# A token list built in bf16, a rotated loop body on VectorE, and moved weight splits in a two-layer expert kernel on one core

## The reference

```
x = soft_moe(x)                      # x = c @ slot_out: each token is a mix of 32 slots
logits = x @ w_gate;  noise_scale = log1p(exp(x @ w_noise))
noisy = logits + noise_scale * noise
top2 = two largest of noisy;  top2_w = softmax over the two
for e in range(E):
    for k in range(2):
        mask = top2[:, k] == e
        h = maximum(x[mask] @ w1[e], 0)
        out[mask] += top2_w[mask, k] * (h @ w2[e])
```

## Time and profile before

| | us |
|---|---|
| median of 3 runs | 1197.89 (1194.05 to 1198.15) |
| the profiled execution | 1196.62 |
| its span, first to last instruction | 1194.8 |
| mean granted PE clock | 0.843 of full speed |

### The profile page before, as it was taken

How to read it: one execution, slowest core, us unless ns; L and a number is a source line. 1 busy time by engine, 2 the same in 40 slices (tenths; PEclk the granted TensorE clock), 3 DMA queues, 4 the chain that set the end, 5 groups by cost and what they waited for, 6 DMA issues and landing times.

```text
span 1194.8 us, 18812 instructions
## 1 busy us (share of the span) xinstructions
PE 958.0 (80%) x5371; PEld 741.2 (62%) x5371; DVE 885.5 (74%) x1882; ACT 414.0 (35%) x758; POOL 666.7 (56%) x817
## 2 busy tenths in 40 slices
PE   4778887888877878787877787857669999999896
PEld 3666665666666666666666675215357877777785
DVE  7999999999999999999999983025444434443432
ACT  3444444444444444444444431110322212221220
POOL 2777777777777777777777751004024444443433
PEclk7888788777788788888788878966779999998998
DMA  9811011011011011011011006999305434423333
GB/s 353 335 41 42 1 42 41 0 41 41 0 41 41 0 41 41 0 41 41 0 41 41 0 1 228 380 421 425 145 10 109 89 55 108 108 29 37 37 38 37
DMA packets 21583, 105.15 MB, mean 88 GB/s; under 512 B 2944, under 2 KB 4016, under 8 KB 12464
## 3 DMA queue, kind: packets, MB, share of 16 engines
q1 hardware_dynamic: 13696, 84.55, 18.1%
q0 software_dynamic: 7136, 11.22, 7.6%
q10 hardware_dynamic: 720, 9.00, 2.0%
HBM read 88.40 MB, written 16.09 MB: 87 GB/s over the span
## 4 chain that ended last, share of the span: by engine, by line
issue 39%; PE 27%; DVE 26%; DMA 4%; DVEq 2%; ACT 1%; POOL 0%; POOLq 0%; SPq 0%; PEldq 0%
PE psum L738 11%; DVE arena L904 9%; DVE arena L900 8%; PE psum L743 5%; DVE arena L893 5%; DMA arena<-w_soft 2%; DMA arena<-xs_rows,arena 2%; PE psum L727 2%; PE psum L698 1%; PE psum L641 1%; PE psum L712 1%; PE psum L534 1%; PE psum L688 1%; DVE h_lo L1139 1%; DVE arena L919 1%
## 5 line engine op out<-in xcount | busy, mean ns | idle before, releaser
L900 DVE MATCH_REPLACE8 arena<-arena 128x576 f32<-128x576 f32 x432 | 316.6, 739 | 0.0
L904 DVE MAX8 arena<-arena 128x8 f32<-128x576 f32 x432 | 303.8, 743 | 0.0
L501 PE MATMUL psum<-arena 128*128 128x128 f32 x576 | 130.2, 367 | 150.3 <-POOL arena L1190 150.2
L1184 POOL TENSOR_SCALAR arena<-arena 128x576 bf16<-128x576 f32 x142 | 244.5, 1731 | 6.6
L486 PE MATMUL psum<-arena 128*128 128x288 f32 x576 | 222.5, 550 | 4.6 <-DMA arena<-qkv 4.6
L514 PEld LDWEIGHTS psum<-arena 128*128 128x128 f32 (+3 forms) x1600 | 193.4, 182 | 30.1 <-issue 3.5
L514 PE MATMUL psum<-arena 128*128 128x65 f32 (+3 forms) x1600 | 207.5, 271 | 0.9 <-ACT arena L782 0.9
L501 PEld LDWEIGHTS psum<-arena 128*128 128x128 f32 x576 | 82.5, 180 | 183.0 <-POOL arena L1190 155.8
L486 PEld LDWEIGHTS psum<-arena 128*128 128x128 f32 x576 | 153.2, 280 | 53.6 <-DMA arena<-qkv 4.6
L1190 POOL TENSOR_TENSOR arena<-arena 128x576 f32<-128x576 f32 x142 | 178.5, 1278 | 0.0
L781 ACT COPY arena<-psum 128x512 f32<-128x512 f32 x144 | 84.2, 585 | 231.3 <-PE psum L502 231.3
(11 more groups left out here) (173 smaller groups left out, 971.4 us busy)
## 6 DMA issues: line engine op xcount, KB each, us to landing
weights<-w_soft SPq DMA_DIRECT2D x21, 1024.0 KB, 16.9
arena<-qkv SPq DMA_DIRECT2D x15, 1189.0 KB, 5.3
weights<-w_top SPq DMA_DIRECT2D x12, 1024.0 KB, 27.4
arena<-w_soft SPq DMA_DIRECT2D x11, 1024.0 KB, 11.6
weights<-w_top SPq DMA_DIRECT2D x3, 2048.0 KB, 21.8
weights<-w_top ACTq DMA_DIRECT2D x3, 2048.0 KB, 8.0
out<-arena SPq DMA_DIRECT2D x1, 4864.0 KB, 18.9
arena<-w_top SPq DMA_DIRECT2D x4, 1024.0 KB, 27.8
```

Of the source, the lines that this page charges most:

```text
L501: nc.tensor.transpose(bank(4 + t % 2, P, c * P), src[:, c * P:(c + 1) * P], ident)
L900: nc.vector.match_replace(work[t % 2], m8[t % S_SLOTS][:, 8 * r - 8:8 * r], src, NEG) \
L904: nc.vector.max(m8[t % S_SLOTS][:, 8 * r:8 * r + 8], work[t % 2]) \
L1184: nc.gpsimd.tensor_scalar(keep[t % 2], s_sb[t % S_SLOTS], m8[t % S_SLOTS][:, TOPK - 1:TOPK], None, ALU.is_ge) \
```

## The change

What it does:
- **The list** is built from bf16 one-hot matrices, exact for the small whole numbers in it, by 36 single-pass matmuls with 94 columns: 47 that add up which of the 36 blocks a row is in, and 47 that add up (partition - 128), made by ACT. POOL makes the first 47, DVE the compare (`col_hot`) and all of `onehot` in three parts. A few DVE operations turn the two sums into a row index and an output row for each place; `list_i` holds both.
- **Tokens from the list**: the 33rd word of a row is gone. An output row is numbered by partition and block rather than by token, and the host puts the rows in the order of tokens at the end. The scatter takes its rows from the list's second word; the copies L1128 and L1147 and the counters `x_free` and `tok_set` go. `fetch` copies both words ahead of the scatter.
- **The gate weights** are worked out earlier on DVE, and POOL instead of DVE multiplies the rows by them.
- **Loop body on DVE rotated**: y of tile i - 1 is taken out at the start of tile i's body. `w2_low(e + 2)` thereby stands between c_low of an expert's last tile and y of that tile.
- **Weight splits** are made in halves; ACT's `w2_high` runs one expert further ahead; `w2_low(1)` stands behind `c_low(1)`, ahead of the first y.
- **G stacks**: eight stacks use six pairs of banks; experts 6 and 7 are taken out only after expert 0's tiles; PE's first f_trans waits for the first six.
- **Bounds**: each engine loads all nine at once ahead of the loop.

The diff, cut to its core (constants, semaphores and layout are left out):

```diff
-        G_BANKS = [(3, 4), (0, 5)]
+        G_BANKS = [(3, 4), (0, 5), (3, 4), (0, 5), (1, 2), (6, 7), (3, 4), (0, 5)]
...
+        def tile_bounds(eng):
+            return [eng.value_load(tab[0:1, e:e + 1], min_val=min(e, 1), max_val=TILES) for e in range(E + 1)]
...
             def g_stack(e):
                 pe.wait_ge(g_lo, 2 * (e // 4) + 2)
-                if e >= 2:
-                    pe.wait_ge(g_ev[0], e - 1)
-                    pe.wait_ge(g_ev[1], e - 1)
+                if e in (2, 3, 6, 7):
+                    last_user = max(n for n in range(e) if G_BANKS[n] == G_BANKS[e])
+                    pe.wait_ge(g_ev[0], last_user + 1)
+                    pe.wait_ge(g_ev[1], last_user + 1)
                 for x in range(2):
                     for n, part_ in enumerate((gq_hi, gq_lo)):
                         first = (1 - n) * SL
-                        last = nc.tensor.matmul(bank(G_BANKS[e % 2][x]), pick[:, e % 4, first:first + P],
+                        last = nc.tensor.matmul(bank(G_BANKS[e][x]), pick[:, e % 4, first:first + P],
                                                 part_[:, x * BANK:(x + 1) * BANK], start=(n == 0), stop=(n == 1))
                     last.then_inc(g_rep, 1)
 
             g_group(0)
 
-            pe.wait_ge(hot_hi, 1)
+            pe.wait_ge(hot_act, 1)
+            pe.wait_ge(hot_pool, 1)
             for a in range(PICKS):
-                if a % 14 == 0:
-                    pe.wait_ge(*((hot_dve, a // 14 + 1) if a < 28 else (hot_pool, 1)))
-                last = nc.tensor.matmul(bank(B_X, COLS), onehot[:, a, :], hi_hot[:, a, :],
+                if a % 12 == 0:
+                    pe.wait_ge(hot_dve, a // 12 + 1)
+                last = nc.tensor.matmul(bank(B_X, 2 * COLS), onehot[:, a, :],
+                                        hi_hot[:, a, :, :].rearrange("p v q -> p (v q)"),
                                         start=(a == 0), stop=(a == PICKS - 1))
             last.then_inc(list_ps, 1)
             pe.wait_ge(pick_set, 1)
@@ -714,11 +715,14 @@
                 last.then_inc(f_t, 1)
 
             pe.wait_ge(rt_ready, 1)
-            pe.wait_ge(idx_ready, 1)
+            bounds = tile_bounds(pe)
+            pe.sem_inc(f_y, 1)
+            pe.wait_ge(g_ev[0], 6)
+            pe.wait_ge(g_ev[1], 6)
             f_trans(16)
             for e in range(E):
-                t0, t1 = first_tile(pe, e), end_tile(pe, e)
-                pe.wait_ge(w_lo, e + 1)
+                t0, t1 = bounds[e], bounds[e + 1]
+                pe.wait_ge(w_lo, 2 * e + 2)
                 pe.wait_ge(g_ev[0], e + 1)
...
-                nc.scalar.copy(w2_hi[e % 4], w2t_of(e % 4)).then_inc(w_hi, 1)
+                for f in (0, FC // 2):
+                    nc.scalar.copy(w2_hi[e % 4][:, f:f + FC // 2, :], w2t_of(e % 4)[:, f:f + FC // 2, :]).then_inc(w_hi, 1)
 
...
             nc.scalar.copy(pick, more[:, M_PICK:MW].rearrange("p (q w) -> p q w", q=4)).then_inc(pick_set, 1)
-            act.wait_ge(rows_set, 2)
-            act.dma_start(xs_dram[0:2 * N, :].rearrange("(p a) r -> p (a r)", a=PICKS), rows_f).then_inc(tabled, 16)
+            act.wait_ge(hot_set, 1)
+            nc.scalar.activation(hi_hot[:, :, 1, :], col_hot, ACT.Copy, scale=cst[:, C_BACK:C_BACK + 1]).then_inc(hot_act, 1)
+            act.wait_ge(rows_set, 1)
+            act.dma_start(xs_dram[0:ROWS, :].rearrange("(p a) r -> p (a r)", a=PICKS),
+                          rows_f).then_inc(tabled, 16)
             g_high(0)
             for e in range(4):
                 g_out(e)
             g_high(1)
             w2_high(0)
-            for e in range(4, E):
+            for e in range(4, 6):
                 g_out(e)
             w2_high(1)
...
+            bounds = tile_bounds(act)
             c_high(1)
...
-                if e < E - 2:
-                    w2_high(e + 2)
+                if e == 0:
+                    g_out(6)
+                    g_out(7)
+                    w2_high(2)
+                if e < E - 3:
+                    w2_high(e + 3)
...
+            link(nc.vector.tensor_scalar(small[5], small[4], 1.0, 1e-9, ALU.add, ALU.add))
+            link(nc.vector.reciprocal(small[5], small[5]))
+            nc.vector.tensor_tensor(small[6], small[4], small[5], ALU.mult).then_inc(gate_set, 1)
 
             dve.wait_ge(sp_, 10)
...
-            row_v = r_key.rearrange("p t e -> p (t e)")[:, PICKS:2 * PICKS]
-            link(nc.vector.tensor_copy(tile_f, tile_i))
-            link(nc.vector.scalar_tensor_tensor(low_of, tile_f, -float(P), pos, ALU.mult, ALU.add))
-            nc.vector.tensor_tensor(row_v, cst[:, C_ROW:C_ROW + PICKS], low_of, ALU.subtract).then_inc(low_set, 1)
+            link(nc.vector.tensor_copy(tile_b, tile_i))
+            link(nc.vector.scalar_tensor_tensor(low_b, tile_b, -float(P), pos, ALU.mult, ALU.add))
+
+            def spread(a, first, n, w):
+                return a[:, first:first + n].unsqueeze(2).broadcast_to([P, n, w])
+
+            nc.vector.tensor_tensor(col_hot, iota_b[:, 0:COLS].unsqueeze(1).broadcast_to([P, PICKS, COLS]),
+                                    spread(tile_b, 0, PICKS, COLS), ALU.is_equal).then_inc(hot_set, 1)
+            for n in range(3):
+                nc.vector.tensor_tensor(onehot[:, 12 * n:12 * n + 12, :],
+                                        iota_b.unsqueeze(1).broadcast_to([P, 12, P]),
+                                        spread(low_b, 12 * n, 12, P), ALU.is_equal).then_inc(hot_dve, 1)
 
             link(nc.vector.tensor_copy(tab[:, 0:E + 1], tiny[:, 24:33]))
             link(nc.vector.tensor_scalar(ti[:, 0:1], tiny[:, 32:33], 1.0, None, ALU.add))
             nc.vector.tensor_scalar(tab[:, E + 1:E + 2], ti[:, 0:1], 1, None, ALU.logical_shift_right) \
                 .then_inc(rt_ready, 1)
...
             def w2_low(e):
-                dve.wait_ge(w_hi, e + 1)
-                nc.vector.tensor_tensor(w2_lo[e % 4], w2t_of(e % 4), w2_hi[e % 4].bitcast(F32), ALU.subtract) \
-                    .then_inc(w_lo, 1)
+                for n, f in enumerate((0, FC // 2)):
+                    dve.wait_ge(w_hi, 2 * e + n + 1)
+                    nc.vector.tensor_tensor(w2_lo[e % 4][:, f:f + FC // 2, :], w2t_of(e % 4)[:, f:f + FC // 2, :],
+                                            w2_hi[e % 4][:, f:f + FC // 2, :].bitcast(F32), ALU.subtract) \
+                        .then_inc(w_lo, 1)
 
             g_low(0)
+            dve.wait_ge(list_ps, 1)
+            got_a, got_p = rt_all[4][:, 0:COLS], rt_all[4][:, COLS:2 * COLS]
+            nc.vector.memset(list_f, 0.0)
+            link(nc.vector.tensor_copy(rt_all[4][:, 0:2 * COLS], bank(B_X, 2 * COLS)))
+            link(nc.vector.scalar_tensor_tensor(v_row, got_p, float(PICKS), got_a, ALU.mult, ALU.add))
+            nc.vector.tensor_scalar(list_i[:, :, 0], v_row, float(ROWS), None, ALU.add).then_inc(idx_ready, 1)
+            link(nc.vector.tensor_scalar(v_back, got_a, float(TT), -float(TT), ALU.is_ge, ALU.mult))
+            link(nc.vector.tensor_tensor(v_back, v_back, got_a, ALU.add))
+            link(nc.vector.scalar_tensor_tensor(v_back, got_p, float(TT), v_back, ALU.mult, ALU.add))
+            link(nc.vector.tensor_scalar(v_empty, got_p, 0.0, cst[:, C_LOW:C_LOW + 1], ALU.is_equal, ALU.mult))
+            nc.vector.scalar_tensor_tensor(list_i[:, 3:COLS, 1], v_back[:, 0:COLS - 3], float(N), v_empty[:, 0:COLS - 3],
+                                           ALU.add, ALU.add).then_inc(idx_ready, 1)
             for e in range(4):
                 g_out(e)
             g_low(1)
             w2_low(0)
-            for e in range(4, E):
+            for e in range(4, 6):
                 g_out(e)
-            w2_low(1)
 
             def c_low(need):
                 dve.wait_ge(f_cs, need)
                 nc.vector.tensor_tensor(cs[64:P, :], bank(B_X, P)[64:P, :], cs[64:P, :].bitcast(F32), ALU.subtract) \
                     .then_inc(f_c, 1)
 
-            def tok_in(need):
-
-                dve.wait_ge(x_ready, need)
-                nc.vector.tensor_copy(tok_next, x_in[:, SL:ROW].bitcast(I32)).then_inc(x_free, 1)
-
-            dve.sem_inc(f_yc, 1)
+            def y_out(i):
+                nc.vector.tensor_copy(y_ring[:, bass.ds((i + 1) % 2 * D, D)], bank(B_Y)).then_inc(f_yc, 1)
+
+            bounds = tile_bounds(dve)
             c_low(1)
-            tok_in(16)
+            w2_low(1)
             for e in range(E):
-                t0, t1 = first_tile(dve, e), end_tile(dve, e)
...
+                t0, t1 = bounds[e], bounds[e + 1]
                 with dve.Fori(t0, t1) as i:
-                    side = i % 2
+                    dve.wait_ge(out_free, i + 1)
+                    dve.wait_ge(f_y, i + 1)
+                    y_out(i)
                     for x in range(2):
                         dve.wait_ge(f_hc, 2 * i + x + 1)
                         nc.vector.scalar_tensor_tensor(
@@ -1142,24 +1154,19 @@
```

(66 more changed lines are left out.)

111 lines of the change are left out of this document (42 added, 69 removed).

## The result

The changed kernel takes 1157.65 us (median of 4 runs, 1156.36 to 1161.86) against 1196.59 for the kernel before beside it (4 runs, 1194.05 to 1198.15). The ratio is 0.9683, 95% interval 0.9651 to 0.9714. The prediction was 1166.5 with a range of 1151 to 1182. The profiled execution took 1157.69 us, 38.9 less than the one of before, and its span is 1155.9 instead of 1194.8.

The account below looks back on a forecast made before the run. Bound by a serial head (808 to 878 us), then a 40-tile loop with TensorE full, plus 29.3 us of stalls at expert changes. Savings of 20.0 (head), 9.9 (loop), 1.3 (tail) sum to 31.2: 1166.5 us, range 1151 to 1182.

Parts of the forecast that it names:

- Rows on GpSimd, 1.0: Head, list: GpSimd multiplying token rows beside VectorE's router operations costs 1.0 us, bounds 0 and 2.5.
- col_hot at 1.95, bf16 at the rate of f32: Head, list: VectorE's compare takes 1.95 us, not halved in bf16 because its second operand is broadcast.
- GpSimd's product waits for all of `onehot`, 825.2: Head, list: GpSimd's product waits until onehot's three parts end at 821.4, ending at 825.2; other end 820.0.
- rival (a): Head, list: GpSimd isn't held or slips between; list ends at 822.7, 5.1 us more gained, 1161.4; chance 0.20.
- List matmuls 108 ns, bounds 82 and 216: Head, list: 36 bf16 matmuls at 108 ns each, 3.9 us, ending the list at 829.1.
- The rest of the head: Stacks, splits, bounds loads and first y copy after the list; first big matmuls at 857.9, 20.0 us earlier.
- Changes behind experts 1 to 5, 14.0: Loop: gather held until w2_low ends, 2.0 us stall plus 0.8 of lower clock, five times: 14.0 us.
- rival (b): Loop: gathers not held by w2_low; experts 1 to 5 cost 0.2 each, 13.8 us less, 1152.7; chance 0.12.
- Rival (d): Loop: fetch awaits scatter's landing, tiles lengthen above 5.8 us landing; slower than before; earlier landing within 4.5; chance 0.04.
- (c): Loop: changes of expert stay as dear as before, 29.3 us; 9.9 more, 1176.4; chance 0.18.
- (e): Small or no gain: GpSimd rows 2.5, matmuls 216 ns, dear bounds and expert changes; 1187 to 1190; chance 0.05.
- The tail, -1.3: After the last matmul: GpSimd's index copy and VectorE's last token copy go, saving 1.3 us, bounds 0 and 1.6.

Follow-up runs that it names:

- w2_whole: Changed kernel with each weight split in one instruction instead of halves, on VectorE and ScalarE: 1182.10 us.
- load_late: Changed kernel with loads of second weights of experts 4 to 7 issued two tiles later, by SyncE instead of ScalarE: 1157.69 us.
- fetch_free: Changed kernel with GpSimd's fetch and copy of y waiting for the scatter before the last, not the last: 1157.56 us.
- gather_first: Changed kernel with the gather issued ahead of the scatter in GpSimd's loop: 1202.76 us.
- best3: Changed kernel with w2_high(2), y_out(0) earlier; gather before scatter; fetch not awaiting last scatter; GpSimd's list product on VectorE; VectorE bounds per expert: 1145.62 us.
- hot_dve: Changed kernel with GpSimd's product of the column hots moved to VectorE, behind the first part of onehot: 1157.30 us.

## Why the prediction was right, and where its terms were off

The direction, the order of the parts and the head step by step held; 8.9 us were missing. That the loop came out no further off than 8.8 us is in part luck: its largest term, 14.0 us of stalls at five changes, came to 0.9, and some 5 us of late landings, for which no term stood, made up a third of that. By its steps:

- **Rows on GpSimd, 1.0.** L1054 and L1058 took 0.85 and 0.93 us, 0.46 and 0.17 for the same operations before: 1.15. Right.
- **col_hot at 1.95, bf16 at the rate of f32.** 1.92: right. The Trainium skill, "VectorE: DVE Perf Modes", section "Mode 2×_1P — pack two bf16 into one 32-bit read", asks for a step of 1 or -1, which the broadcast operand hasn't, and 1.92 us against 2.01 in f32 agrees.
- **GpSimd's product waits for all of `onehot`, 825.2.** Wrong, and the first of the mis-sized terms. It waited for the first part alone and finished at 822.86 in a profile that ran 2.1 late, that is 820.8, near the other end given (820.0); the price was paid by VectorE, 2.6 us. So 24 of the 36 matmuls ran beside `onehot`, and only 1.1 us of them stood behind it instead of 3.9. The list ended at 827.3 - 2.1 = 825.2 instead of 829.1: 3.9 us, all of the head's surplus of 3.7. That is rival (a), by its "slips between", at three quarters of its 5.1: it left out that VectorE's next part would wait in turn. The Trainium skill, "SBUF — State Buffer", section "Who interferes with whom", says that the order of issue decides who blocks. The trace agrees: issued ahead of the second part, GpSimd stretched it from 1.75 to 4.57 us.
- **List matmuls 108 ns, bounds 82 and 216.** 57 at the higher clock and 93 at the lower, 81 in the mean, at the lower bound. Only the last twelve counted.
- **The rest of the head.** c_high and c_low were predicted at 851.6 and 852.6, and by the two shifts (+2.1, -3.9) would be at 849.8 and 850.8: measured 849.46 and 850.63. `w2_low(1)` 4.49, y_out(0) at 855.48, L742 at 856.31: step by step as written. The bounds loads lay beside `w2_low(0)` but for 0.9 us.
- **Changes behind experts 1 to 5, 14.0.** Here the sum was furthest off. "The gather, held the same way, starts when w2_low ends": it is through 1.0 behind the end of the first half, 2.25 us sooner, and L713 waits for it only behind expert 2 (0.48 us, beside a load). The row it rested on the earlier trace rows was of a split in one instruction of 4.42 us, and w2_whole shows that with such a one the forecast stall comes: 9.0 and 8.8 us where no load is beside it, against 8.85 forecast, and 12.5 to 12.9 where one is. In the changed kernel the five changes cost 0.9 in all, 0.5 of it behind expert 2. That is about rival (b)'s price, though not its mechanism: the gather *is* held under a tensor_tensor. The Trainium skill infers in the same section ("Who interferes with whom") that descriptor generation isn't stalled by one; by this case that doesn't hold for these indirect transfers.
- **What took its place, not foreseen:** late landings in other tiles, 3.5 us behind the loads of weights and 1.3 in the last tile but one (an empty tile's gather). With 0.8 of lower clock in the first tile, the 0.9 above and small remainders it is 6.6 us over the loop; with expert 0's 4.0 (predicted 5.4, by the mechanism named, ScalarE's 7.4 us of splits; 1.6 of it clock that load_late hasn't) the loop's stalls are 10.6 instead of 19.4.
- **Rival (d), landing of a scatter 4.5 at most.** Wrong: the scatter of 918.74 landed after 5.0 us and the fetch that waits for it began after 5.6 (924.33), 0.2 below the point at which a tile grows. fetch_free shows that it still didn't decide, gather_first what it would have cost. The chance of 0.04 was small for so thin a margin.
- **Rivals (c) and (e)** fell with the changes of expert and the 93 ns: neither the clock at each change nor the list was as dear as they had it.
- **The tail, -1.3.** The last gather does start 0.6 sooner behind the last matmul, but lands in 4.6 us instead of 2.7. Of these 1.9 us some 0.7 go with its following the scatter by 1.9 instead of 2.66 us, as in the full tiles (3.4); the other 1.2 only the empty tiles' gathers have, and no run tests why. Net +1.4.

## What to carry to other kernels

Split a long VectorE operation that runs beside GpSimd's transfers into pieces without changing its total: what GpSimd loses is the rest of the piece it meets. Issue the transfer that somebody waits for first, and check then that nothing in its queue waits for the landing of the other: either edit alone gave nothing or made it slower. And before a difference between two profiles is explained, count it from a common point: here 4.4 us of it was chance from ahead of everything that differed, and single tiles differed by 1.2 to 1.6 us by the clock alone.

## What the runs showed of the hardware

- An indirect gather, 1.08 us of GpSimd alone, took 2.15 under halves of 2.25 and 4.28 under one of 4.42. A scatter, 1.59 alone, took 2.99 and 4.87. A copy of 128x2 words, 0.18 alone, took up to 2.15 us in the same way (gather_first).
- Its data land about 5.3 us after the start of the scatter ahead of it, whether it follows by 2.7 us (landing 2.6) or by 1.9 (3.4); ahead of the scatter it lands in 2.5. It looks as if its data queue behind the scatter's; that was not tested by itself.
- Beside a load of 2 MB a gather lands in 5.0 to 7.4 us (7.4 in best3), in both places tried for the load; one that started 5.4 us behind the load's issue (897.68) landed in 3.5.
- A wait of TensorE can put the clock of the next tile at a mean of 0.80 and cost 1.6 us again, but its length doesn't settle it. After 2.31 us the next tile was at 0.80 in the changed kernel and at 1.00 in fetch_free; in load_late it was at 0.80 after 1.57 and 1.29 us and at 1.00 after 1.58 and 1.20.
- Two VectorE instructions and one of GpSimd with two SBUF inputs each took turns by the order of issue: 1.75 and 4.57 us for the two parts of `onehot` round a product of 4.47, and 1.75 for each part without it (hot_dve).
